# Gated attention and experts on one core: first weight set laid out by steps, its low parts made by VectorE, fold split five and three, prologue placed anew

## What is computed

```
for t in range(S):
    state = alpha[:, :, t, :, None] * state + einsum('bhd,bhe->bhde', k[:, :, t], v[:, :, t])
    y[:, :, t] = einsum('bhd,bhde->bhe', q[:, :, t], state)
x = y as (3072, 384)
x = ((x @ w1) * (x @ w2)) @ w3 @ w_out          # w1, w2: 384x1024, w3: 1024x1024, w_out: 1024x384
p = probs / (probs.sum(-1) + 1e-9)
out = sum over e of p[:, e] * (relu(x @ e_w1[e]) @ e_w2[e])
```

## Time and profile before

| | |
|---|---|
| median of 3 runs | 1240.86 us (1240.52 to 1241.27) |
| the profiled execution | 1242.98 us |
| its span, first to last instruction | 1241.2 us |
| TensorE busy in the span | 1230.0 us (99%) |
| VectorE, ScalarE, GpSimd busy | 446.3, 284.2, 185.2 us |
| mean granted clock of TensorE | 0.996 of full |
| first product of the first tile | 70.46 us |

### The profile page before, as it was taken

One profiled execution on the slowest core, in us unless ns is written; L12 is line 12 of the kernel. 1 busy time (PEld: TensorE's weight loads), 2 busy tenths in 40 slices (PEclk: granted clock), 3 DMA queues, 4 the chain that ended last, 5 costly groups with the idle time before them and its releaser, 6 DMA issues.

```text
span 1241.2 us, 18697 instructions
## 1 busy us (share of the span) xinstructions
PE 1230.0 (99%) x7774; PEld 1118.3 (90%) x7774; DVE 446.3 (36%) x846; ACT 284.2 (23%) x530; POOL 185.2 (15%) x157
## 2 busy tenths in 40 slices
PE   8999999999999999999999999999999999999999
PEld 5589999999999989999898999999899999989898
DVE  4875855855852122222222222212222222222222
ACT  2423333333332421111111111111111111111111
POOL 1522322322221630000000000000000000000000
PEclk9999999999999999999999999999999999999999
DMA  9612432332322431111141111103111111222200
GB/s 270 209 41 67 127 88 69 117 97 69 110 74 109 140 142 51 51 51 51 51 153 51 51 51 51 51 31 126 49 51 51 51 51 51 77 76 76 77 16 35
DMA packets 41317, 99.62 MB, mean 80 GB/s; under 512 B 3360, under 2 KB 13344, under 8 KB 40736
## 3 DMA queue, kind: packets, MB, share of 16 engines
q1 hardware_dynamic: 41248, 98.63, 24.5%
HBM read 82.10 MB, written 14.16 MB: 78 GB/s over the span
## 4 chain that ended last, share of the span: by engine, by line
PE 97%; DMA 2%; DVE 1%; SPq 0%; issue 0%; DVEq 0%
PE bank L865 27%; PE bank L867 27%; PE bank L866 27%; PE score_banks L865 3%; PE score_banks L866 3%; PE score_banks L867 3%; PE bank L901 2%; PE bank L1047 1%; PE score_banks L922 1%; PE bank L911 1%; DMA inputs<-akq 1%; PE bank L1062 1%; DMA wo_sb<-w_out 1%; PE score_banks L887 1%; PE score_banks L874 1%; DVE suffix L636 0%
## 5 line engine op out<-in xcount | busy, mean ns | idle before, releaser
L706 DVE SCALAR_TENSOR_TENSOR h_lo<-bank,h_hi 128x512 fp32r<-128x512 f32 x192 | 132.7, 691 | 617.9 <-ACT h_hi L507 617.9
L507 ACT ACTIVATE h_hi<-bank 128x512 fp32r<-128x512 f32 x192 | 115.0, 599 | 663.9 <-PE bank L867 663.9
L867 PE MATMUL bank<-x_hi,we_lo 128*128 128x512 f32 x576 | 228.1, 396 | 0.0
L866 PE MATMUL bank<-x_lo,we_hi 128*128 128x512 f32 x576 | 227.1, 394 | 0.0
L865 PE MATMUL bank<-x_hi,we_hi 128*128 128x512 f32 x576 | 226.4, 393 | 0.0
L865 PE MATMUL bank<-we_hi,h_hi 128*128 128x384 f32 x576 | 192.4, 334 | 0.0
L867 PE MATMUL bank<-we_hi,h_lo 128*128 128x384 f32 x576 | 192.4, 334 | 0.0
L866 PE MATMUL bank<-we_lo,h_hi 128*128 128x384 f32 x576 | 192.4, 334 | 0.0
L408 POOL TENSOR_TENSOR we_lo<-we_raw,we_hi (+1 forms) x48 | 60.9, 1290 | 529.7 <-ACT we_hi L468 529.7
L867 PEld LDWEIGHTS bank<-x_hi,we_lo 128*128 128x128 f32 x576 | 108.2, 188 | 24.9
L865 PE MATMUL bank<-x,wb_hi 128*128 128x384 f32 x384 | 130.0, 339 | 0.0
(11 more groups left out here) (87 smaller groups left out, 1479.1 us busy)
## 6 DMA issues: line engine op xcount, KB each, us to landing
x_hi<-x_hi_spill SPq DMA_DIRECT2D x24, 768.0 KB, 4.9
x_lo<-x_lo_spill SPq DMA_DIRECT2D x24, 768.0 KB, 6.5
inputs<-akq SPq DMA_DIRECT2D x24, 672.0 KB, 5.4
we_raw<-wset SPq DMA_DIRECT2D x4, 3072.0 KB, 10.2
values<-v_rows SPq DMA_DIRECT2D x24, 256.0 KB, 5.6
x_hi_spill<-x_hi_out SPq DMA_DIRECT2D x8, 576.0 KB, 3.4
x_lo_spill<-x_lo_out SPq DMA_DIRECT2D x8, 576.0 KB, 4.9
w_sb<-w_t SPq DMA_DIRECT2D x16, 256.0 KB, 11.9
```

The costliest lines, as they stand in the source:

```text
L507: act.activation(h_hi[:, s % 2, :], bank[s % 2][:, :], ACT.Relu).then_inc(h_hi_ready, 1)
L706: dve.scalar_tensor_tensor(out=h_lo[:, s % 2, :], in0=bank[s % 2][:, :], scalar=0.0, in1=h_hi[:, s % 2, :], op0=ALU.max, op1=ALU.subtract) ...
L866: pe.matmul(dst, left[0], right[1], start=False, stop=False)
L867: return pe.matmul(dst, left[1], right[0], start=False, stop=last)
```

## The change

- The first weight set is laid out by steps in HBM and in SBUF: for each step f the three blocks of w1 and the three of w2, 768 columns together. `pieces_of(f)` gives the pieces of 512 columns that complete step f: 2, 1, 2, 1, 2, 1, 2, 1 pieces.
- Its low parts are made by VectorE (`piece_low`), none by GpSimd. The pieces of steps 0 and 1 (three) come in the prologue, on ScalarE behind `x0_high(0, 1)` and on VectorE behind `fold_low(5)`. The other nine come in steps 0 to 5 of the first tile, at the start of each step s, for step s + 2, on both engines. `up1(0, s, 0)` waits for its own pieces only, where it waited for half and then for all of the set.
- `FOLD_FIRST` goes from 4 to 5: first loop of five column blocks, second of three; the first part of w3's load has 640 columns and not 512. Column block 5 now waits for the first low part of the fold (it takes its bank).
- On TensorE visit 0 comes one row earlier (k = 6), keys 1 after k = 5, keys 2 at the end of the first loop (k = 7) instead of at n = 5 of the second; the rest of the second loop's table is moved up, with keys 4 at its very end (n = 23).
- VectorE's `take(b, c)` is cut into `advance` (decay, state, mask) and `x0_low`; the advance of the next chunk now comes before the first low part of the fold and the x0 low part. In the last stretch `x0_low(0, 2)` comes before the advance of chunk 3.
- ScalarE does `x0_high(0, 0)` before the fold's copies; `turn_keys(0, 4)` goes behind `fold_high(7)`.

```diff
-FOLD_FIRST = FT // 2
+FOLD_FIRST = 5
+        def pieces_of(f):
+            return range(-(-2 * KT * P * f // PIECE), -(-2 * KT * P * (f + 1) // PIECE))
...
@@ gpsimd
             scale_queries(0, 2)
-            for q in range(3):
-                pieces_low(0, q)
             scale_queries(0, 3)
-            for q in range(3, PIECES // 2):
-                pieces_low(0, q)
             scale_queries(0, 4)
@@ scalar
+            def first_piece_high(i):
+                at = slice(i * PIECE, (i + 1) * PIECE)
+                act.wait_ge(part_loaded[i * PARTS // PIECES], 16)
+                act.activation(wb_hi[:, at], wb_raw[:, at], ACT.Copy).then_inc(piece_hi, 1)
...
+                    if beside and b == 0 and s + 2 < FT:
+                        for i in pieces_of(s + 2):
+                            first_piece_high(i)
                     if following:
                         a_copy(b, s + 1)
...
             turn_keys(0, 1)
-            for f in range(FOLD_FIRST):
+            x0_high(0, 0)
+            fold_high(0)
+            fold_high(1)
+            turn_keys(0, 2)
+            for f in range(2, FOLD_FIRST):
                 fold_high(f)
-            x0_high(0, 0)
             check(0, 2)
-            turn_keys(0, 2)
-            pieces_high(0, 0)
-            fold_high(4)
             x0_high(0, 1)
-            pieces_high(0, 1)
-            pieces_high(0, 2)
+            for f in range(2):
+                for i in pieces_of(f):
+                    first_piece_high(i)
             check(0, 3)
             turn_keys(0, 3)
             fold_high(5)
-            pieces_high(0, 3)
-            pieces_high(0, 4)
             x0_high(0, 2)
-            pieces_high(0, 5)
             fold_high(6)
-            turn_keys(0, 4)
             check(0, 4)
             fold_high(7)
+            turn_keys(0, 4)
@@ vector
+            def piece_low(i):
+                at = slice(i * PIECE, (i + 1) * PIECE)
+                dve.wait_ge(piece_hi, i + 1)
+                dve.tensor_tensor(wb_lo[:, at], wb_raw[:, at], wb_hi[:, at], ALU.subtract).then_inc(piece_lo, 1)
+            def advance(b, c):
+                if c >= 1:
+                    decay_state(b, c)
+                if c < CHUNKS - 1:
+                    add_state(b, c)
+                mask(b, c)
...
+                    if beside and b == 0 and s + 2 < FT:
+                        for i in pieces_of(s + 2):
+                            piece_low(i)
                     if second:
                         prepare_clamp(*second)
...
-            add_state(0, 0)
-            mask(0, 0)
+            advance(0, 0)
             prepare_factors(0, 1)
             prepare_clamp(0, 2)
             prepare_suffixes(0, 2)
             prepare_factors(0, 2)
-            take(0, 0)
-            for f in range(FOLD_FIRST):
+            advance(0, 1)
+            fold_low(0)
+            x0_low(0, 0)
+            for f in range(1, FOLD_FIRST):
                 fold_low(f)
             prepare_clamp(0, 3)
             prepare_suffixes(0, 3)
-            take(0, 1)
+            advance(0, 2)
             prepare_factors(0, 3)
-            fold_low(4)
+            x0_low(0, 1)
             fold_low(5)
+            for f in range(2):
+                for i in pieces_of(f):
+                    piece_low(i)
             prepare_clamp(0, 4)
             prepare_suffixes(0, 4)
-            take(0, 2)
+            x0_low(0, 2)
+            advance(0, 3)
             prepare_factors(0, 4)
@@ tensor
+                    if isinstance(b, int) and b == 0 and s < FT:
+                        pe.wait_ge(piece_lo, pieces_of(f).stop)
...
-                    cols = slice((which * KT + k) * FF + f * P, (which * KT + k) * FF + (f + 1) * P)
+                    cols = slice(((2 * f + which) * KT + k) * P, ((2 * f + which) * KT + k + 1) * P)
...
-            first_beside = {3: (turn_keys, 0), 4: (first_visit, 0), 6: (turn_keys, 1), 7: (visit, 0)}
-            second_beside = {5: (turn_keys, 2), 8: (visit, 1), 15: (turn_keys, 3), 18: (visit, 2), 27: (turn_keys, 4)}
+            first_beside = {3: (turn_keys, 0), 4: (first_visit, 0), 5: (turn_keys, 1), 6: (visit, 0), 7: (turn_keys, 2)}
+            second_beside = {4: (visit, 1), 10: (turn_keys, 3), 14: (visit, 2), 23: (turn_keys, 4)}
...
-                if k == 0 and f > FOLD_FIRST:
-                    pe.wait_ge(fold_lo, f - FOLD_FIRST)
+                if k == 0:
+                    pe.wait_ge(fold_lo, FOLD_BANKS[f] + 1)
...
             pe.wait_ge(fold_lo, FT - 2)
-            pe.wait_ge(piece_lo, PIECES // 2)
             up1(0, 0, 0, True)
             pe.wait_ge(fold_lo, FT - 1)
-            pe.wait_ge(piece_lo, PIECES)
             up1(0, 0, 1, True)
```

More of the change, by code:

```diff
@@ L460, in _ @@
         def _(act):
+            def first_piece_high(i):
+                at = slice(i * PIECE, (i + 1) * PIECE)
+                act.wait_ge(part_loaded[i * PARTS // PIECES], 16)
+                act.activation(wb_hi[:, at], wb_raw[:, at], ACT.Copy).then_inc(piece_hi, 1)
             def pieces_high(n, q):
                 for i in range(2):
-                    if isinstance(n, int) and n == 0:
-                        act.wait_ge(part_loaded[(2 * q + i) * PARTS // PIECES], 16)
-                    else:
-                        act.wait_ge(set_loaded, 16 * n)
+                    act.wait_ge(set_loaded, 16 * n)
                     at = piece_at(q, i)
@@ L707, in h_low @@
                                          in1=h_hi[:, s % 2, :], op0=ALU.max, op1=ALU.subtract).then_inc(h_lo_ready, 1)
-            def take(b, c):
-                first = chunk_behind(b, c)
-                if first:
-                    if first[1] >= 1:
-                        decay_state(*first)
-                    if first[1] < CHUNKS - 1:
-                        add_state(*first)
-                    mask(*first)
-                x0_low(b, c)
+            def piece_low(i):
[8 more added lines that the diff above has]
+                mask(b, c)
             def bilinear(b, beside=True, last_batch=False):
@@ L732, in bilinear @@
                     if chunk:
-                        take(*chunk)
+                        if chunk_behind(*chunk):
+                            advance(*chunk_behind(*chunk))
+                        x0_low(*chunk)
                     if last_batch and beside and s == FLAG_STEP:
@@ L1167 @@
                for k in range(KT) for q in range(2) for i in range(ODD)]
+    wset0 = np.stack([by_rows(w[x0_rows]).reshape(P, KT, FT, P) for w in (moe_w1, moe_w2)], axis=1)
+    wset0 = np.ascontiguousarray(wset0.transpose(0, 3, 1, 2, 4).reshape(P, WSET))
     arrays = {
@@ L1174 @@
         "w_out": by_rows(moe_w_out),
-        "wset0": weight_set(moe_w1[x0_rows], moe_w2[x0_rows]),
+        "wset0": wset0,
         "probs": by_rows(moe2_domain_probs),
```

## The result

The changed kernel takes **1236.07 us** (median of 7 runs, 1235.57 to 1236.40); the kernel before takes 1240.86 us (7 runs, 1239.04 to 1243.14). The ratio is 0.9961, 95% interval 0.9949 to 0.9973: faster by 0.39%, 4.8 us. Forecast were 1235.3 us and a gain of 5.5. One later run of the kernel before (1339.01 us, granted clock 0.85) lay in a slow state of the chip and is left out of every figure.

The account below looks back on a forecast made before the run. TensorE was taken as the bound, with only its idle and half-clock time before the first tile winnable. Gain 6.4 us there less 0.9 in the tile, 5.5 off the 1240.86 us median: 1235.3 us, range 1229.5 to 1239.0.

Parts of the forecast that it names:

- The bound: Whole kernel: TensorE never waits from the first tile on; only its idle and half-clock time before 70.46 us can be won.
- The 12.4 us: Before the first tile: 6.8 us of TensorE idle time and 5.6 us of half clock, there to be had.
- what is won in the span I take off the median, 2.1 us below the profiled time: Final conversion: the forecast gain in the profiled span, 5.5 us, subtracted whole from the unprofiled median, 1240.86 us.
- Low parts from GpSimd to VectorE: Prologue and first tile: slow scans end (4.05 and 3.0 us off VectorE), twelve subtractions of 0.62 us are added.
- The lock: VectorE and GpSimd's shared ports: an exclusive lock, so a moved subtraction is held for the rest of any GpSimd product met.
- rival (d): First tile: VectorE becomes the bound through subtractions held by GpSimd; 10.4 us lost against 6.4 won, 1244.9 us; chance 0.08.
- Fold five and three: Prologue: 5.2 us of fold products moved forward; wait for w_out part 3 becomes 1.4 us instead of 2.03, no clock fall.
- What is late next: Prologue's end: chunk 4's load lands at 55.4 us, TensorE idles 3.5 us, clock halves (1.85 us); gain 6.4 us.
- rival (b): Prologue's end: the load of chunk 4 doesn't bind, landing by 51.9 us; tile starts at 58.7, 1230.0 us; chance 0.10.
- The new wait of 0.6 us before keys 2: End of the first loop: TensorE reaches keys 2 at 36.5 us, the mask of chunk 1 ends at about 37.1.
- In the first tile: First tile: one TensorE wait of 0.9 us for step 3's weights, bounds 0 and 2; then VectorE stays ahead.
- lie in idle time: First tile: ScalarE's nine copies, 0.57 us each, fit its idle time; where that is gone, one or two lengthen the path.

Follow-up runs that it names:

- low_on_dve: Kernel before with all twelve low parts made by VectorE, still all in front of the tile, nothing else changed; 1238.25 us, ratio 0.9979.
- pool_low: Changed kernel with the low parts made by GpSimd again, at the same places in its order; 1235.53 us, ratio 0.9958.
- fold4: Changed kernel with the fold split four and four again and the visit tables of before; 1236.37 us, ratio 0.9968.
- high_early: Changed kernel with ScalarE making the first tile's nine high copies in the prologue instead; 1233.65 us, ratio 0.9949.
- before_again: Kernel before, unchanged, run once more for a second trace; 1239.70 us (one run).
- move_later: Kernel before with the x0 move of chunk 1 issued behind the load of chunk 5 instead of chunk 4; 1240.85 us, ratio 0.9994.
- low_dve_move_later: Kernel before with all low parts on VectorE and the x0 move of chunk 1 behind the load of chunk 5; 1237.68 us, ratio 0.9979.

## Why the prediction was right

The forecast of the time held because two wrong terms of it, the prologue and the first tile, went opposite ways; that was luck. The parts one by one:

**The bound.** Right: TensorE's idle and half-clock time in front of the tile, and nothing else, was to be won. The 12.4 us were of one execution, though; the second trace of before has 3.3 us less of it. The step "what is won in the span I take off the median, 2.1 us below the profiled time" was wrong in kind: part of those 2.1 us was the very thing that the change takes away. Of the gain of the traces it must go off again, as it did.

**Low parts from GpSimd to VectorE.** The subtraction: forecast 0.62 us, measured 0.60 from start to start (74.92 to 75.52). The scans: 1.61 and 1.37 us as forecast. That this frees the prologue: right, but low_on_dve and pool_low show what the prediction didn't separate. The hold ends as well if most of the low parts leave the prologue and GpSimd keeps them (pool_low, 1235.5 us). The engine alone is worth 2.8 us, the place alone (with the rest of the change) 5.5, both together 4.8 and 5.0 in two groups of runs; the last two are one value within their intervals.

**The lock.** SBUF — State Buffer of the Trainium skill (section SBUF: two separate sides) has the shared pair as an exclusive lock. The case agrees as far as it goes: scans beside GpSimd's low parts in the tile are 0.2 us longer on average, those under GpSimd's unbroken work three to four times as long. A subtraction is held too: in low_on_dve one takes 1.53 us, as long as the rest of the GpSimd product that it met and then 0.55 us, as the prediction had it. The changed kernel made few such meetings (its longest of twelve takes 0.80 us), so the price that rival (d) put on them did not come. Subtractions that read the fold's bank (`wp_lo`) were not held: two at 53.46 us in the trace of before take 0.99 us beside a product from 53.61 to 54.87 us.

**Fold five and three.** Forecast an idle time of 1.4 us at the third load; there was none in the trace of after, and fold4 lost at most 0.4 us. The step that failed is the scaling of 14.69 us by bytes: this load takes up to 2 us more or less in the same kernel.

**What is late next.** The wrong term. Forecast: landing at 55.4, a wait of 3.5 us, the clock halved, tile at 62.2, in all a gain of 6.4 us. Measured: landing at 52.09, keys at 58.57 without a wait, clock full, tile at 58.91, 11.55 us. From landing to key product it was 6.4 us as forecast (52.09 to 58.43); it was the landing that was 3.3 us off: 1.3 us because the parts were issued at 38.50 and not at 39.8, 2.0 us because they and the load took 13.6 and not 15.6 us. That is rival (b), which had 0.10. The step that failed is that the same bytes in front were taken to need the same time; the small transfers beside them were not at the same times. With it three of the signs named beforehand stayed out: the wait of 2 to 4 us before chunk 4's keys, the half clock behind it, and the first product near 62.2 us. The new wait of 0.6 us before keys 2 is not in this trace either (0.37 to 0.38 us in three of the later ones).

**In the first tile.** The other wrong term. The first wait was right in place, engine and size (0.94 us at 75.75, forecast 0.7 to 0.9 at 16 us after the start, 16.8 measured). "From then on VectorE is ahead (11.3 against 12.4) and nothing more is lost" was wrong: 3.3 us in place of 0.9. The sum of VectorE's work was right (11.3 us a pair, and 11.5 in high_early); what was left out is in whose order the copies stand that the subtractions wait for. That ScalarE's nine copies "lie in idle time" is true for ScalarE, but VectorE waits for them in order, behind ScalarE's check, 2.6 and 3.0 us. Rival (d), VectorE as the bound, came true as a mechanism, through that wait and not through GpSimd, at a third of its price.

**Together.** Forecast 6.4 - 0.9 = 5.5 us off the median. Measured 11.55 - 3.3 = 8.3 us between the two traces, of which 1.0 us went at the end of the execution and 2.6 us were the distances of the two executions from their medians. So the prologue gave 5.2 us more than forecast, the tile took 2.4 us more, and 3.6 us went where the forecast had nothing: 5.5 + 5.2 - 2.4 - 3.6 = 4.7 us, against the 4.8 of the medians. The closeness of 1235.3 to 1236.07 us says little for the reasoning.

## What to carry to other kernels

Work moved onto an engine that has time for it must also be handed its operands in time: look at where in its engine's order their producer stands, not only whether it is idle. The high copies belonged in the prologue, where ScalarE had time, and with that and two low parts moved into a gap the kernel is at 1232.5 to 1233.1 us, some 3 us faster than the changed kernel. Where stalls and the clock decide, take a second trace of the kernel before pricing them: here two executions of one kernel differ by 3.3 us in the place that the change was for.

## What the runs showed of the hardware

- The clock after a wait is not settled by the wait's length: after 2.01 us (before) and 2.12 us (low_on_dve) it fell and eight product records took 4.45 us; after 2.10 us (before_again) it did not and they took 2.76. It fell as well after 2.03 and 1.81 us (before), 2.78 us (before_again), 2.79 and 2.05 us (move_later). Of TensorE's waits between products of up to 1.76 us (the longest in low_dve_move_later) none had a fall behind it in any trace.
- The time of a load in the middle of others varies with what goes on beside it: 11.1 us or 8.4 us for the same 672 KB with the same 3 MB in front, a 96 KB move and GpSimd's work being what differed. With GpSimd silent the move alone made 10.3 or 8.4 us, one trace each.
- A VectorE subtraction of 128x512 float32 from SBUF takes 0.60 to 0.62 us from start to start where nothing holds it, and one that started 0.3 us into a GpSimd product of 1.27 us took 1.53 us (low_on_dve).
- VectorE scans of 112x128 take 1.37 and 1.60 us for four alone, and 5.4 and 4.6 to 5.6 us beside unbroken GpSimd products of 128x512 (before, before_again, move_later).
